# Two-way attention and two expert layers on one core: where the side work stands in a step of TensorE

## The chip, the cores and the metric

The kernel runs on one core of a Trainium2 chip. Its time is the device time of one execution in microseconds (us); lower is better. A median over several executions is given, and one more execution was profiled.

## What is computed

```python
# attention: x (8,8,512,64), state (8,8,32,64), batch and head first
a = softmax(scale * x @ state.T);  xread = a @ state
a2 = softmax(scale * state @ x.T); sread = a2 @ x
x = concat([xread, sread], axis=2)        # -> (4352, 512) rows
# first layer, w_in (512,2048), w_out (2048,512)
h = x @ w_in
x = (h - tanh(h)) @ w_out
# second layer, 8 experts, each token goes to its best one, w1 (8,512,1024), w2 (8,1024,512)
probs = softmax(x @ w_gate);  e = argmax
out[token] = probs[e] * (relu(x[token] @ w1[e]) @ w2[e])
```

## The kernel before

**The dense part.** The function `attention_moe_kernel` runs over 9 tiles t: one of 512 rows for each of the B = 8 batches (the xread rows), and a last one of 256 rows (all the sread rows). Each tile has FC = 16 chunks f of the 2048 hidden columns. A step c = 16 t + f on TensorE is: `first_product(c)`, the product h of chunk c, which writes one of two PSUM banks; `second_product(c - LAG)` with LAG = 3, the product with w_out that adds the chunk of three steps ago into the four banks of x2 (one for each 128 rows); and `side_work(c)`. All products are split in a high and a low part of the operands, so h takes 6 matmuls of 512 columns (r and three pairs of parts), and the product of x2 takes 12 (four blocks of rows, three pairs of parts). Nearly all matmuls are issued by the helper `mm` on line 1002, so the rows of the trace tell them apart by their operands: `ps<-A,G` is h, `ps<-wout,g_hi` and `ps<-wout,g_lo` are the product of x2, `ps<-win,stT` is `make_G`.

The text calls the side work of step f "side f", and the end of the h product of step f "the end of h f".

**The side work** is what the next tiles need and what the last tile leaves: 
- side 0: `turn_sread` and, from tile 2 on, `ranks(t - 2)`. 
- sides 1 to 3: `make_G`, the quarters 1 to 3 of G = state times w_in of this tile, which the h products of f = 4 on read. Side 1 waits for `ranks_read` from tile 2 on.
- sides 4 to 6: `turn`, `turn` and `gate_logits` of the tile before; side 7: `turn_logits`.
- sides 7 to 11: `attn_stage(t + 1, 0..4)`, side 12: `make_G(t + 1, 0)`, sides 13 to 15: `attn_stage(t + 1, 5..7)`. Only where a tile t + 1 below 8 follows, so 7 times.

Each side stage writes the two PSUM banks P0 and P1 (called P01 together). ScalarE (ACT) copies them out, for G also VectorE (DVE) takes the low part from them (`make_G_lo`, line 815), and the next side stage waits for that.

**The other engines.** Each of them has an order written out by hand, by step. ACT in step c: `tanh_of(c)` (lines 599 to 601, three passes over h), `g_hi_of(c - 1)` (line 607), in step 2 `y_copies` of the four x2 banks of the last tile (line 624), and then its share of the side work (such as `make_G_hi`, line 588). DVE in step c: `h_less_tanh(c)` (lines 897, 901, 904, 906), then its share. GpSimd (POOL) makes `g_lo` (line 480), and in steps 12 and 13 runs `shift` (line 451) and `normalize` (line 456) ahead of the `g_lo` of its own step. All wait in order: nothing passes a waiting instruction on its engine.

**The chain of the state softmax.** In tile t, for tile t + 1: side 11 writes the scores, ACT copies them (`S1_copied`), DVE takes the maxima (`max_states`), POOL subtracts them (`shift`, in step 12 behind `g_lo` of chunk 11), ACT takes the exponential (`exp_states`, line 577), DVE sums (`sums`), POOL multiplies (`normalize`, in step 13 behind `g_lo` of chunk 12), and then side 14 (`attn_stage(t + 1, 6)`, line 1046) turns the result on TensorE; it waits for `a_ready`.

The semaphore of h chunk c is waited for by ACT; h c + 2 waits for `g_made` of chunk c, since it takes its bank.

**Behind the dense part** comes the table of tokens by expert and a loop over tiles of 128 tokens, each with its expert's weights. The change doesn't touch it.

Of the kernel before, what the change touches and what calls it, by code (L numbers as in the profile page):

```python
# [21 lines left out]
def attention_moe_kernel(nc, x, state, w_in, w_out, w_gate, w1, w2, out):  # L22
# [50 lines left out]
    with ExitStack() as ctx:  # L73
# [244 lines left out]
        def width(t):  # L318
            return S if t < B else SR
# [680 lines left out]
        def _(pe):  # L1000
            def mm(o, l, r, start, stop):
                return nc.tensor.matmul(o, l, r, start=start, stop=stop)  # L1002
# [56 lines left out]
            def make_G(b, nb):  # L1059

                for pr in range(PAIRS):
                    for r in range(2):
                        rows = slice(D * r, D * (r + 1))
                        last = mm(ps[NS * pr:NS * (pr + 1), 6 + r, :], stT[rows, pr, NS * r:NS * (r + 1)],
                                  win[rows, pr, nb * 512:(nb + 1) * 512], True, True)
                last.then_inc(G_done, 1)

            def turn_sread(b):
                pe.wait_ge(sreadN_made, b + 1)
                nc.tensor.transpose(P0[:, 0:P], sreadN[:].rearrange("p r d -> p (r d)"), ident[:]).then_inc(sread_turned, 1)  # L1070

            def turn(t, i):
                pe.wait_ge(y_copied, C * t + i + 1)
                for k in range(K):
                    last = nc.tensor.transpose(ps[:, 6 + i % 2, P * k:P * (k + 1)], x2[:, i, P * k:P * (k + 1)], ident[:])  # L1075
                last.then_inc(x2_turned, 1)

            def gate_logits(t):

                pe.wait_ge(x2T_copied, C * (t + 1))  # L1080
                for k in range(K):
                    last = mm(P0[NS * k:NS * (k + 1), :], wg[:, k, :], x2T[:, :, k, :], True, True)
                last.then_inc(logits_done, 1)

            def turn_logits(t, bank, n):
                pe.wait_ge(LT_copied, t + 1)
                for i in range(n):
                    last = nc.tensor.transpose(bank[:, P * i:P * (i + 1)], LT[:, P * i:P * (i + 1)], ident[:])
                last.then_inc(LT_turned, 1)

            def ranks(tp, n):
                pe.wait_ge(onehot_made, tp + 1)
                mm(P1[:, 0:n * E], before[:], onehot[:, 0:n, :].rearrange("p t e -> p (t e)"), True, False)
                mm(P1[:, 0:n * E], ones[:], seen[:, 0:n, :].rearrange("p t e -> p (t e)"), False, True
                   ).then_inc(ranks_done, 1)

            def first_product(c):
                t, f = c // FC, c % FC
                if c >= 2:
                    pe.wait_ge(g_made, c - 1)  # L1100
                o = PH[c % 2][:, 0:width(t)]
                fs = slice(f * P, (f + 1) * P)
                if t < B:
                    if f == 0:
                        pe.wait_ge(A_lo_made, t + 1)
                    if f % 4 == 0:
                        pe.wait_ge(G_lo_made, NB * t + f // 4 + 1)
                    hi, lo = A_hi[t % 2], A_lo[t % 2]
                    for r in range(2):
                        for q, (l, m) in enumerate(((G_hi, hi), (G_hi, lo), (G_lo, hi))):  # L1110
                            last = mm(o, l[:, r, fs], m[:, r, :], r == 0 and q == 0, r == 1 and q == 2)
                else:
                    if f == 0:
                        pe.wait_ge(sread_copied, B)
                    for k in range(K):
                        last = mm(o, win[:, k, fs], sread[:, k, :], k == 0, k == K - 1)
                last.then_inc(h_done, 1)

            def second_product(c):
                t, f = c // FC, c % FC  # L1120
                n = width(t)
                pe.wait_ge(g_lo_made, c + 1)
                if t == 0 and f % 2 == 0:
                    wait_split(pe, f // 2)
                for i in range(n // P):
                    if f == 0 and t > 0:
                        pe.wait_ge(y_copied, C * (t - 1) + i + 1)
                    ts = slice(i * P, (i + 1) * P)
                    for q, (l, r) in enumerate(((g_hi, wout_hi), (g_hi, wout_lo), (g_lo, wout_hi))):
                        last = mm(PY[i], l[:, c % GR, ts], r[:, f, :], f == 0 and q == 0, f == FC - 1 and q == 2)  # L1130
                    if f == FC - 1:
                        last.then_inc(y_done, 1)
                if f < FC - 1:
                    last.then_inc(g_used, 1)
                else:
                    pe.sem_inc(g_used, 1)

            def side_work(c):
                t, f = c // FC, c % FC
                if f == 0:  # L1140
                    if t == 0:
                        attn_stage(0, 7)
                    elif t < B:
                        turn_sread(t)
                    if 2 <= t < B:
                        ranks(t - 2, C)
                elif f < NB and t < B:
                    if f == 1:
                        if t == 0:
                            pe.wait_ge(sreadN_made, 1)  # L1150
                        else:
                            pe.wait_ge(sread_copied, t + 1)
                        if t >= 2:
                            pe.wait_ge(ranks_read, t - 1)
                    else:
                        pe.wait_ge(G_lo_made, NB * t + f)
                    if t == 0:
                        pe.wait_ge(win_loaded[f], 16)
                    make_G(t, f)
                if t == 0 and f == 5:  # L1160
                    pe.wait_ge(G_lo_made, NB)
                    turn_sread(0)
                if t > 0:
                    if f == 4:
                        if t < B:
                            pe.wait_ge(G_lo_made, NB * (t + 1))
                        else:
                            pe.wait_ge(ranks_read, t - 1)
                            pe.wait_ge(logits_made, t - 1)
                        turn(t - 1, 0)  # L1170
                        turn(t - 1, 1)
                    elif f == 5:
                        for i in (2, 3):
                            pe.wait_ge(x2T_copied, C * (t - 1) + i - 1)
                            turn(t - 1, i)
                    elif f == 6:
                        gate_logits(t - 1)
                    elif f == 7:
                        turn_logits(t - 1, P1, C)
                if f == 11 and t >= B - 1:  # L1180
                    pe.wait_ge(logits_made, t)
                    ranks(t - 1, C)
                if t + 1 < B:
                    if f == 7 and t == 0:
                        pe.wait_ge(sread_copied, 1)
                    if f == 8 and t > 0:
                        pe.wait_ge(logits_made, t)
                    if 7 <= f < 12:
                        attn_stage(t + 1, f - 7)
                    elif f == 12:  # L1190
                        pe.wait_ge(S1_copied, t + 2)
                        make_G(t + 1, 0)
                    elif f > 12:
                        attn_stage(t + 1, f - 8)
# [17 lines left out]
            pe.wait_ge(gate_w_loaded, 16)  # L1212
            for c in range(FC * (B + 1)):
                first_product(c)
                if c >= LAG:
                    second_product(c - LAG)
                side_work(c)
            for c in range(FC * (B + 1) - LAG, FC * (B + 1)):
                second_product(c)

# [113 lines left out]
```

## Time and profile before

| | before |
|---|---|
| median of 3 executions | 1280.41 us |
| lowest, highest | 1278.49, 1280.99 us |
| the profiled execution, its own time | 1278.91 us |
| its span | 1277.2 us |
| mean granted TensorE clock | 0.978 |
| busy: TensorE matmul (and weight loads), ACT, DVE, POOL | 95% (75%), 50%, 58%, 41% |
| busy time of TensorE matmul | 1213.2 us |

The span runs from the first to the last instruction of the profiled execution; its own time lies 1.7 us above it. The share of busy time is an average: the dense part takes the stretch from about 40 us to 750 us, the experts that from about 798 us to the end.

### The profile page before, as it was taken

How to read it: one execution, taken by the hardware profiler on the slowest of the kernel's cores; microseconds unless marked ns; L12 is line 12 of the kernel's file. 1: busy time of each engine (PE TensorE's matmuls, PEld its weight loads, DVE VectorE, ACT ScalarE, POOL GpSimd, SP SyncE). 2: the span in 40 equal slices, each digit the busy share in tenths (PEclk: the TensorE clock that was granted, in tenths of full speed). 3: DMA queues.
4: the chain of work that ended last, by engine and by line, in shares of the span. 5: the costliest groups of instructions: out<-in, count | busy, mean ns of one | idle time of the engine just before them, and what ended most of it. 6: DMA issues, size and time to landing. Idle time of an engine off the chain costs nothing.

```text
span 1277.2 us, 20438 instructions
## 1 busy us (share of the span) xinstructions
PE 1213.2 (95%) x6740; PEld 961.1 (75%) x6741; DVE 745.3 (58%) x1018; ACT 632.8 (50%) x1088; POOL 522.3 (41%) x379
## 2 busy tenths in 40 slices
PE   6799999999999999999999965999999999999995
PEld 4577777877777777777778744888888888888884
DVE  4698788788887888878887765050500023282400
ACT  3556666666665666566654532333333333333332
POOL 3244234244243442434424232454544455555543
PEclk8899999999999999999999987999999999999998
DMA  8200301103003020020200206142411123353311
GB/s 261 67 20 1 67 3 47 23 1 67 3 9 61 1 67 3 1 67 1 77 24 4 96 18 222 42 133 82 141 66 41 41 89 123 113 168 102 104 35 37
DMA packets 74655, 80.71 MB, mean 63 GB/s; under 512 B 52063, under 2 KB 52063, under 8 KB 73570
## 3 DMA queue, kind: packets, MB, share of 16 engines
q1 hardware_dynamic: 55506, 59.80, 16.3%
q0 software_dynamic: 7568, 20.03, 4.7%
q10 hardware_dynamic: 11520, 0.09, 0.5%
q8 instruction: 37, 0.61, 0.2%
q14 instruction: 24, 0.20, 0.1%
HBM read 61.70 MB, written 19.49 MB: 64 GB/s over the span
## 4 chain that ended last, share of the span: by engine, by line
PE 80%; DVE 6%; POOL 5%; ACT 3%; DMA 3%; issue 2%; ACTq 0%; POOLq 0%; SPq 0%; DVEq 0%
PE ps L1002 72%; PE ps L1281 3%; POOL g_lo L480 2%; PE ps L1244 1%; DMA sread<-x_rows,take 1%; POOL xx L456 1%; POOL xx L451 1%; PE ps L1075 1%; PE ps L1019 1%; DVE u L904 1%; DVE u L897 1%; PE ps L1046 1%; ACT th L600 1%; DMA take<-expert_tokens 1%; DVE u L901 1%
## 5 line engine op out<-in xcount | busy, mean ns | idle before, releaser
L1002 PE MATMUL ps<-W,A 128*128 x1872 | 448.6, 395 | 2.8 <-ACT A L715 1.3
L1002 PEld LDWEIGHTS ps<-W,A 128*128 128x128 f32 x1872 | 347.4, 189 | 73.5 <-issue 3.8
L480 POOL TENSOR_TENSOR g_lo<-u,g_hi 128x512 fp32r<-128x512 f32 (+1 forms) x144 | 186.8, 1297 | 435.7 <-ACT g_hi L607 404.2
L1002 PE MATMUL ps<-wout,g_hi 128*128 128x512 f32 x1088 | 339.2, 393 | 0.4 <-POOL g_lo L480 0.4
L1002 PEld LDWEIGHTS ps<-wout,g_hi 128*128 128x128 f32 x1088 | 204.2, 188 | 43.8 <-POOL g_lo L480 1.1
L1002 PE MATMUL ps<-A,G 128*128 128x512 f32 x768 | 210.3, 409 | 4.4 <-issue 2.5
L1002 PE MATMUL ps<-wout,g_lo 128*128 128x512 f32 x544 | 212.4, 390 | 0.0
L889 DVE CAST W<-xn 128x1024 fp32r<-128x1024 f32 x28 | 21.5, 769 | 303.6 <-PE ps L1002 302.7
L904 DVE COPY_PREDICATED u<-big,th 128x512 f32<-128x512 uint8 (+1 forms) x144 | 179.7, 1248 | 23.4 <-DVE u L901 23.1
L1002 PEld LDWEIGHTS ps<-A,G 128*128 128x128 f32 x768 | 135.7, 189 | 67.9 <-issue 39.8
L599 ACT ACTIVATE u<-ps 128x512 f32<-128x512 f32 (+1 forms) x144 | 82.7, 574 | 118.1 <-PE ps L1002 97.9
L897 DVE SCALAR_TENSOR_TENSOR u<-u 128x512 f32<-128x512 f32 (+1 forms) x144 | 109.8, 763 | 48.8 <-ACT u L599 48.8
L1002 PEld LDWEIGHTS ps<-wout,g_lo 128*128 128x128 f32 x544 | 102.1, 188 | 22.3
L709 ACT ACTIVATE th<-ps 128x1024 f32<-128x1024 f32 x39 | 40.0, 1027 | 142.2 <-PE ps L1002 142.2
L901 DVE SCALAR_TENSOR_TENSOR u<-u,ps 128x512 f32<-128x512 f32 (+1 forms) x144 | 94.8, 658 | 24.0 <-ACT big L601 14.1
L721 ACT ACTIVATE sread<-ps,put 128x512 f32<-128x512 f32 x39 | 26.8, 687 | 159.3 <-PE ps L1002 150.9
L501 POOL TENSOR_TENSOR A<-LT,A 128x512 fp32r<-128x512 f32 x40 | 54.3, 1358 | 122.1 <-ACT LT L705 122.1
L506 POOL TENSOR_TENSOR A<-u,A 128x1024 fp32r<-128x1024 f32 x39 | 97.8, 2509 | 4.6 <-ACT u L716 4.0
L906 DVE TENSOR_TENSOR u<-ps,u 128x512 f32<-128x512 f32 (+1 forms) x144 | 95.3, 662 | 4.9
L607 ACT CAST g_hi<-u 128x512 fp32r<-128x512 f32 (+1 forms) x144 | 87.5, 608 | 7.2 <-DVE u L906 7.2
L495 POOL DMA_INDIRECT out_rows<-sread,put x39 | 47.1, 1208 | 100.4 <-ACT sread L721 96.0
L601 ACT ACTIVATE big<-ps 128x512 uint8<-128x512 f32 (+1 forms) x144 | 83.3, 579 | 0.0
(154 smaller groups left out, 1211.9 us busy)
## 6 DMA issues: line engine op xcount, KB each, us to landing
xn<-in_moe_w SPq DMA_DIRECT2D x32, 512.0 KB
xn<-in_x SPq DMA_DIRECT2D x32, 256.0 KB
x_rows<-xx SPq DMA_DIRECT2D x8, 1024.0 KB
spare<-in_moe_w SPq DMA_DIRECT2D x16, 512.0 KB
sp<-in_moe_w SPq DMA_DIRECT2D x16, 512.0 KB
win<-in_moe_w_in SPq DMA_DIRECT2D x4, 1024.0 KB, 11.2
Araw<-in_moe_w_out SPq DMA_DIRECT2D x6, 512.0 KB, 6.2
spare<-in_moe_w_out SPq DMA_DIRECT2D x2, 512.0 KB, 6.0
```

The source lines that it names most:

```text
L480: nc.gpsimd.tensor_tensor(g_lo[:, c % GR, 0:n], u[:, c % 2, 0:n], g_hi[:, c % GR, 0:n], ALU.subtract).then_inc(g_lo_made, 1)
L495: nc.gpsimd.indirect_dma_start(out, bass.IndirectOffsetOnAxis(ap=put[:, 0:1], axis=0), y_rows, None, bounds_check=TOK - 1, oob_is_err=Fals ...
L501: nc.gpsimd.tensor_tensor(xe_lo.rearrange("p k s -> p (k s)"), xe_raw, xe_hi.rearrange("p k s -> p (k s)"), ALU.subtract).then_inc(xe_lo_m ...
L506: nc.gpsimd.tensor_tensor(he_lo.rearrange("p k s -> p (k s)"), h_raw, he_hi.rearrange("p k s -> p (k s)"), ALU.subtract).then_inc(he_lo_ma ...
L599: nc.scalar.activation(u[:, c % 2, 0:n], h, ACT.Square, scale=SQ ** 0.5).then_inc(v_made, 1)
L601: nc.scalar.activation(big[:, c % 2, 0:n], h, ACT.Square, scale=0.5 ** 0.5 / SMALL).then_inc(big_made, 1)
L607: nc.scalar.copy(g_hi[:, c % GR, 0:n], u[:, c % 2, 0:n]).then_inc(g_hi_made, 1)
L897: nc.vector.scalar_tensor_tensor(uu, uu, LIN, uu, ALU.add, ALU.mult).then_inc(poly_made, 1)
L901: nc.vector.scalar_tensor_tensor(uu, uu, 1.0, h, ALU.add, ALU.mult).then_inc(near_made, 1)
L904: nc.vector.copy_predicated(uu, big[:, c % 2, 0:n], tt).then_inc(tanh_chosen, 1)
L906: nc.vector.tensor_tensor(uu, h, uu, ALU.subtract).then_inc(g_made, 1)
L1002: return nc.tensor.matmul(o, l, r, start=start, stop=stop)
```

## The change

In the loop over the steps on TensorE, `side_work(c)` is called between `first_product(c)` and `second_product(c - LAG)`, no longer behind both.

```diff
             for c in range(FC * (B + 1)):
                 first_product(c)
+                side_work(c)
                 if c >= LAG:
                     second_product(c - LAG)
-                side_work(c)
             for c in range(FC * (B + 1) - LAG, FC * (B + 1)):
                 second_product(c)
```

The orders of ACT, DVE, POOL and SyncE stay word for word as they are, and so do the number of instructions and what each waits for. Two places of the order on TensorE show what moves. `xx` holds the state softmax, `A` and `G` are the operands of h, `wout`, `g_hi` and `g_lo` those of the product of x2. First, step 14 of a tile, before:

```order
L1002 MATMUL ps<-A,G 128x512 [waits g_made]
L1002 MATMUL ps<-A,G 128x512 x5
L1002 MATMUL ps<-wout,g_hi 128x512 [waits g_lo_made]
...
L1002 MATMUL ps<-wout,g_lo 128x512
L1046 MATMUL ps<-ident,xx 128x128 [waits a2T_copied,a_ready]
L1046 MATMUL ps<-ident,xx 128x128 x7
```

And with the change:

```order
L1002 MATMUL ps<-A,G 128x512 [waits g_made]
L1002 MATMUL ps<-A,G 128x512 x5
L1046 MATMUL ps<-ident,xx 128x128 [waits a2T_copied,a_ready]
L1046 MATMUL ps<-ident,xx 128x128 x7
L1002 MATMUL ps<-wout,g_hi 128x512 [waits g_lo_made]
...
L1002 MATMUL ps<-wout,g_lo 128x512
```

The 12 matmuls of the product of x2 have gone from ahead of side 14 to behind it; between side 13 and side 14 there is still one product of x2, that of the step before.

Second, step 3 of a tile, before, with the wait for the four copied banks of x2 and the one for the last quarter of G:

```order
L1002 MATMUL ps<-A,G 128x512 x5
L1002 MATMUL ps<-wout,g_hi 128x512 [waits y_copied,g_lo_made]
L1002 MATMUL ps<-wout,g_hi 128x512
...
L1002 MATMUL ps<-wout,g_lo 128x512
L1002 MATMUL ps<-win,stT 32x512 [waits G_lo_made]
L1002 MATMUL ps<-win,stT 32x512 x7
```

And with the change:

```order
L1002 MATMUL ps<-A,G 128x512 x5
L1002 MATMUL ps<-win,stT 32x512 [waits G_lo_made]
L1002 MATMUL ps<-win,stT 32x512 x7
L1002 MATMUL ps<-wout,g_hi 128x512 [waits y_copied,g_lo_made]
L1002 MATMUL ps<-wout,g_hi 128x512
...
L1002 MATMUL ps<-wout,g_lo 128x512
```

In step 2 the same move puts the last product into the x2 banks of the old tile, for which ACT's `y_copies` wait, behind `make_G` of quarter 2.

## Rows read from the trace of the kernel before

**Rows 1.** Busy time by stretch: length, then PE, PEld, DVE, ACT, POOL, clock, DMA.

```profile
45.00:90.00 45.00, 39.99 (x214) 29.64 (x214) 40.97 (x45) 26.77 (x51) 18.98 (x11) 1.00 0.21 49
...
289.00:371.00 82.00, 81.84 (x509) 62.36 (x508) 68.41 (x99) 51.99 (x96) 30.50 (x22) 1.00 0.14 27
...
687.00:750.00 63.00, 61.57 (x290) 50.77 (x290) 44.29 (x93) 30.83 (x82) 19.30 (x23) 1.00 0.15 51
```

**Rows 2.** Timeline of TensorE, tile 3, step 14: start, length, instruction, idle before.

```profile
356.84 0.61 PE L1002 MATMUL ps<-wout,g_hi 128*128 128x512 f32 x2
...
359.33 0.39 PE L1002 MATMUL ps<-wout,g_lo 128*128 128x512 f32 x1
359.88 1.09 PE L1046 MATMUL ps<-ident,xx 128*128 128x128 f32 x8 [0.16 <-POOL xx L456]
```

**Rows 3.** Who waited for line 456, us in total and times.

```profile
  PEld ps L1046: 4.1, 7
```

**Rows 4.** Timeline of POOL, tile 3, steps 12 to 14.

```profile
350.19 2.38 POOL L451 TENSOR_TENSOR xx<-xx,m 128x1024 f32<-128x1024 f32 x1
355.77 1.72 POOL L480 TENSOR_TENSOR g_lo<-u,g_hi 128x512 fp32r<-128x512 f32 x1 [3.20 <-ACT g_hi L607]
357.43 2.40 POOL L456 TENSOR_TENSOR xx<-xx,r 128x1024 f32<-128x1024 f32 x1
```

**Rows 5.** Timeline of ACT, tile 3, steps 12 and 13.

```profile
346.73 0.60 ACT L599 ACTIVATE u<-ps 128x512 f32<-128x512 f32 x1 [0.36 <-PE ps L1002]
...
352.60 1.06 ACT L577 ACTIVATE xx<-xx 128x1024 f32<-128x1024 f32 x1 [1.05 <-POOL xx L451]
353.57 0.58 ACT L599 ACTIVATE u<-ps 128x512 f32<-128x512 f32 x1
...
355.00 0.63 ACT L607 CAST g_hi<-u 128x512 fp32r<-128x512 f32 x1
```

**Rows 6.** Timeline of TensorE, tile 1, steps 2 and 3.

```profile
133.19 0.39 PE L1002 MATMUL ps<-wout,g_lo 128*128 128x512 f32 x1
133.51 1.09 PE L1002 MATMUL ps<-win,stT 64*32 64x512 f32 x16
...
138.85 1.09 PE L1002 MATMUL ps<-win,stT 64*32 64x512 f32 x16
```

**Rows 7.** Timeline of ACT, tile 1, step 2.

```profile
132.84 2.07 ACT L624 COPY xx<-ps 128x512 f32<-128x512 f32 x4
134.75 1.08 ACT L588 CAST G<-ps 128x1024 fp32r<-128x1024 f32 x1
```

**Rows 8.** Timeline of DVE, tile 1, step 2.

```profile
135.86 1.23 DVE L815 TENSOR_TENSOR G<-ps,G 128x1024 fp32r<-128x1024 f32 x1
```

**Rows 9.** Timeline of TensorE, tile 3, sides 1, 8 and 13.

```profile
292.77 1.09 PE L1002 MATMUL ps<-win,stT 64*32 64x512 f32 x16
...
328.96 1.04 PE L1019 MATMUL ps<-ident,xn 128*128 128x128 f32 x8
...
354.59 1.03 PE L1040 MATMUL ps<-ident,xx 128*128 128x128 f32 x8
```

**Rows 10.** Timeline of DVE, tile 3: what sides 1, 8 and 13 wait for.

```profile
291.09 0.19 DVE L875 TENSOR_TENSOR score<-ps,region 128x32 f32<-128x32 f32 x1
...
326.19 0.28 DVE L829 TENSOR_REDUCE logits<-ps 128x32 f32<-128x128 f32 x1
...
351.58 1.23 DVE L815 TENSOR_TENSOR G<-ps,G 128x1024 fp32r<-128x1024 f32 x1
```

**Rows 11.** Timeline of TensorE, first tile.

```profile
52.44 1.09 PE L1002 MATMUL ps<-win,stT 64*32 64x512 f32 x16 [3.27 <-DVE G L815]
...
57.77 1.09 PE L1002 MATMUL ps<-win,stT 64*32 64x512 f32 x16
...
76.76 1.67 PE L1002 MATMUL ps<-A,G 128*128 128x512 f32 x6 [0.76 <-DVE u L906]
```

**Rows 12.** Timeline of DVE, first tile, steps 2 and 3.

```profile
56.34 1.22 DVE L815 TENSOR_TENSOR G<-ps,G 128x1024 fp32r<-128x1024 f32 x1
```

## The prediction

> **What bounds the kernel now.** I read four views, in this order. The page's busy time first (the table above): TensorE is busy for 95% of the span and loads weights for 75%. A share over all stages doesn't say what the dense part is worth, so next the busy time by stretch [rows 1]: in a full tile TensorE is busy 81.84 of 82.00 us, in the first tile 39.99 of 45.00 and in the last 61.57 of 63.00. So from 45 to 750 us it sits idle for some 5.0 + 1.4 us in the first and last tile and 0.16 in each of the eight stretches between (1.3): **7.7 us in all**. No order can win more than that there, since the change takes no instruction away. What it can lose is open: each side stage waits for ACT, DVE or POOL, and these waits are hidden now only because they end before TensorE comes to the side. Hence the third view, the timelines around each side: when does what it waits for end, and what would be left if TensorE came sooner? The fourth, who waited for line 456, says which wait already isn't hidden: side 14 waited 7 times, 4.1 us in total on the weight loads [rows 3].
>
> **What moves.** The product of x2 lasts, from its first matmul at 356.84 to its last at 359.33, 11 spacings of 0.227 us; 12 of them are **2.73 us** [rows 2]. It goes from ahead of each side to behind it. From one side to the next the same work stands as before (one h, one product of x2), so nothing changes between sides. But what the sides wait for hangs on the ends of h (ACT's tanh passes come first in its step, then g_hi, DVE and POOL follow), and from the end of an h to a side of the same or a later step there is now one product of x2 less: every side comes 2.73 us sooner against those engines. A wait with slack over 2.73 us, or one that moves along with the side itself, costs nothing; one with slack s costs 2.73 - s; one with no slack costs all of it. Switching between kinds of matmul occurs as often as before (h, side, x2 for x2, side, h), and I cost it at nothing. The h products wait for g_made of two chunks ago; one side and one product of x2 lie in between as before.
>
> I went through all 16 sides of a full tile.
>
> *Side 14 (`a_ready`).* The h of step 12 ends just before 346.73, where ACT's tanh begins [rows 5]. From there to POOL's `shift` at 350.19 there is g_hi and g_lo of chunk 11 in between; `shift` takes 2.38 [rows 4], ACT's exponential stands at 352.60, tanh of step 13 follows at 353.57 and g_hi at 355.00 [rows 5], then POOL's g_lo from 355.77 and `normalize` from 357.43 to 359.83 [rows 4]. Side 14 starts at 359.88 [rows 2], 13.15 us behind the end of h 12. That whole chain is anchored to the end of h 12, and it is longer than what TensorE has to do, so it has no slack: it started 0.23 us later than the usual 0.32 behind the last matmul at 359.33 [rows 2]. Side 14 can't come sooner, and the product of x2 that covered the chain is now behind it. Full price: **2.73 us, 7 times, 19.1 us**. In this is what side 13 waits (its G low part ends at 352.81 [rows 10], side 13 would come at 354.59 - 2.73 = 351.86 [rows 9], so it waits 1.0): both lie ahead of the same fixed point.
>
> *Side 3 (`G_lo_made`).* In step 2 ACT copies the four x2 banks of the old tile, 132.84 to 134.91, and only then quarter 2 of G [rows 7]; DVE takes its low part from 135.86 to 137.09 [rows 8]; side 3 starts at 138.85 [rows 6], a slack of 1.7. Now the last of those banks is done after `make_G`. The end of h 2 is at about 130.84 (2.75 ahead of 133.58, where the last matmul of x2 ends [rows 6]); with the side, 1.11 us, ahead of it, the fourth bank is done at 134.69, its copy takes to about 135.25, the copy of G (1.02) to 136.2, DVE's low part (1.23) to 137.5. Side 3 would come at 138.85 - 2.73 = 136.12. It waits **1.42 us, in tiles 1 to 7: 9.9 us**. If ACT passed these on with no delay, its old time of 137.09 would give 1.0 each.
>
> *Side 1 (`ranks_read`).* DVE reads the ranks at the end of a row of small operations behind its step 0, to 291.28; side 1 starts at 292.77 and would come at 290.04 [rows 9, 10]. With 0.05 for the semaphore: **1.29 us, in tiles 2 to 7: 7.7 us**.
>
> *Side 8 (`logits_made`).* DVE ends the logits at 326.47, side 8 starts at 328.96 and would come at 326.23 [rows 9, 10]: **0.29 us, in tiles 1 to 6: 1.7 us**.
>
> *All others* wait for one ACT copy of the side before. ACT is through with tanh and g_hi some 2.1 us behind the end of h (353.57 to 355.63 [rows 5]) and then copies for 1.0, so it is done 3.2 us after the side began where a side comes every 5.0. Side 12 is the tightest, since ACT takes two exponentials ahead of its copy, by an estimated 0.3 us. Nothing. Side 2 and side 4 gain what sides 1 and 3 wait and stay just clear (0.4 us each). The store of x2 starts with the last copy, and the transposes' copies come as long after it as before: nothing.
>
> *First tile.* No product of x2 stands in steps 0 to 2, so nothing moves there. Side 3 waits for quarter 2's low part, which ends at 57.56 [rows 12]: it starts then, where it now starts at 57.77 [rows 11], but the product of x2 comes behind it, so h 4 is late by 2.5 us. Here DVE is the bound (40.97 busy of 45.00 [rows 1]) and takes up some 1.5 of that. Bounds: 0 (DVE and a DMA set the pace anyway, h 8 waits 0.76 for DVE [rows 11]) and 2.6. I take **1.4**. *Last tile and experts:* sides 4 to 7 and 11 only, with 3 us steps whose copies take under 2.5: nothing. The experts shift as a whole.
>
> **Sum:** 19.1 + 9.9 + 7.7 + 1.7 + 1.4 = 39.8 us. On the profiled execution's own 1278.9 this is 1318.7. The median of the runs shown is 1.5 above that execution, so I predict **1320.2 us**, 3.1% slower.
>
> **The rivals.**
> - *The chains come forward with the sides (faster).* The Trainium skill, Perfetto Trace Analysis, Optimization Strategy, says to find the gap on the engine that matters and to make what it waits for start sooner; this change does start every side stage sooner. As a mechanism: the copies fall in ACT's idle time, POOL's `shift` starts early enough that side 14 no longer waits (0.23 us, 7 times), and the first tile's h products no longer wait for DVE (0.76 and two smaller, 1.7 in all): -3.3 us, 1277.1. It decides if `shift` begins before 350.19 minus 0.23 relative to h 12. Against it: `shift` stands behind g_lo of chunk 11, which hangs on the end of h 12 and not on side 11. 2%. That it all cancels, within 0.2%: 2%.
> - *Only the wait without slack pays.* Sides 1, 3 and 8 depend on sums of durations that DVE and POOL stretch or shorten. If those stay hidden: 19.1 and nothing else, 1299.5. Against it are the slacks of 1.5 to 2.5 in the rows. 9%.
> - *The waits add instead of overlapping.* Side 13's 1.0 us comes on top of side 14's 7 times, and the first tile pays 2.6: 39.8 + 7.0 + 1.2, 1328.4. For it: POOL and DVE hold each other up now and then (g_lo takes 1.72 instead of 1.3 [rows 4]). 11%.
> - *The clock falls after the new waits.* The granted clock was 0.978 on average, so somewhere in the run, outside the dense stretches, it was at the lower of its two levels. If each wait at side 14 cost the next h and x2 (4.1 us) half their speed: 7 more times 4.1, 28.7, 1349. Against it: side 2 of the first tile came after 3.27 us idle and still took 1.09, as everywhere, with a clock of 1.00 in that stretch [rows 1, 11]; only the one at side 3 of the first tile (2.6) is longer than 2.0. [...] 2%.
>
> **How the numbers follow.** The forecast has 74%. The range reaches from just above the case where only side 14 pays to just above the one where waits add: 1304 to 1330, which leaves out the ends, some 15%. What a measurement of this kernel can tell from no change is about 0.2%, 2.6 us. Slower by more: 74 + 9 + 11 + 2 = 96%. Within it 2%, faster 2%.
>
> **What would show it.** In the new profile: side 14 (line 1046) waits for POOL line 456 some 2 us, 7 times, side 13 some 1 us for DVE line 815; `make_G` waits for line 815 in step 3 by some 1.4 us in tiles 1 to 7 and for line 875 in step 1 by 1.3 us in tiles 2 to 7; side 8 waits some 0.3 us for line 829. The busy time of TensorE stays at 1213 us, its clock at 0.98, the tiles 2 to 6 each get 5.7 us longer (2.73 + 1.42 + 1.29 + 0.29), and the experts take as long as now. Tiles no longer than now would prove me wrong: then the chains follow the sides and not the h products. Tiles over 8 us longer would mean a wait that I put down as hidden.

## The result, and the profile after

The changed kernel takes 1325.93 us in the median of 4 executions (1323.43 to 1328.79), the kernel before 1280.12 us beside it. The ratio is 1.036, 95% interval 1.0334 to 1.0387: slower by 45.8 us. The forecast was 1320.2, slower by 39.8.

| | before | after |
|---|---|---|
| the profiled execution, its own time | 1278.91 us | 1323.43 us |
| its span | 1277.2 us | 1321.7 us |
| mean granted TensorE clock | 0.978 | 0.976 |
| busy time of TensorE matmul | 1213.2 us | 1220.1 us |
| share of TensorE, ACT, DVE, POOL | 95, 50, 58, 41% | 92, 47, 57, 39% |

The list of who waited for whom, TensorE alone, in the changed kernel: us in total, times, longest.

```profile
PE ps L1002 <- DVE G L815: 14.1, 9, 3.4
PE ps L1046 <- POOL xx L456: 13.0, 7, 1.9
PE ps L1040 <- DVE G L815: 10.9, 8, 5.2
PE ps L1002 <- DVE score L875: 8.0, 6, 1.3
...
PE ps L1019 <- DVE logits L829: 0.9, 6, 0.2
```

Five sides wait, and they are those of the forecast: sides 3, 14, 13, 1 and 8. Of the nine waits of the first row one was there before (3.35 us, side 2 of the first tile) and one is new and small (0.35 us, side 3 of the first tile); of the eight of the third one was there before (5.2 us, at the start). The timeline of TensorE, between side 13 of tile 2 and side 3 of tile 3, answers to [rows 2, 6, 9]:

```profile
281.98 1.06 PE L1040 MATMUL ps<-ident,xx 128*128 128x128 f32 x8 [0.81 <-DVE G L815]
...
289.02 1.09 PE L1046 MATMUL ps<-ident,xx 128*128 128x128 f32 x8 [1.87 <-POOL xx L456]
...
302.76 1.52 PE L1002 MATMUL ps<-A,G 128*128 128x512 f32 x6
305.61 1.09 PE L1002 MATMUL ps<-win,stT 64*32 64x512 f32 x16 [1.33 <-DVE score L875]
...
309.50 1.52 PE L1002 MATMUL ps<-A,G 128*128 128x512 f32 x6
310.95 1.09 PE L1002 MATMUL ps<-win,stT 64*32 64x512 f32 x16
...
314.84 1.52 PE L1002 MATMUL ps<-A,G 128*128 128x512 f32 x6
317.86 1.09 PE L1002 MATMUL ps<-win,stT 64*32 64x512 f32 x16 [1.49 <-DVE G L815]
```

From side 14 of one tile to side 14 of the next it is 88.35 us here (200.67 to 289.02), where it was 82.30 before (195.29 to 277.59, the same tile): 6.05 us more, and 5.99 to 6.07 in four of the five tiles 2 to 6. That the waits are those of fixed chains is to be seen on POOL, in the same tile:

```profile
278.09 1.30 POOL L480 TENSOR_TENSOR g_lo<-u,g_hi 128x512 fp32r<-128x512 f32 x1 [3.67 <-ACT g_hi L607]
279.34 2.38 POOL L451 TENSOR_TENSOR xx<-xx,m 128x1024 f32<-128x1024 f32 x1
284.92 1.72 POOL L480 TENSOR_TENSOR g_lo<-u,g_hi 128x512 fp32r<-128x512 f32 x1 [3.20 <-ACT g_hi L607]
286.60 2.37 POOL L456 TENSOR_TENSOR xx<-xx,r 128x1024 f32<-128x1024 f32 x1
```

ACT begins tanh of step 12 at 275.87 there:

```profile
275.87 0.60 ACT L599 ACTIVATE u<-ps 128x512 f32<-128x512 f32 x1 [0.57 <-PE ps L1002]
```

Side 14 starts at 289.02, 13.15 us later, to the hundredth what it was [rows 2, 5]. `shift` and `normalize` start 3.47 and 10.73 us behind that tanh, where they started 3.46 and 10.70 behind it. Not one link moved by more than 0.03 us.

One tile is out of line. From side 14 of tile 3 (377.38) to that of tile 4 (467.28) it is 89.90 us. The 8 us behind the two, by stretch (length, then PE, PEld, DVE, ACT, POOL, clock, DMA):

```profile
377.38:385.38 8.00, 8.00 (x91) 6.68 (x92) 4.44 (x6) 2.43 (x5) 1.27 (x1) 0.79 0.00 0
467.28:475.28 8.00, 8.00 (x98) 6.59 (x99) 5.54 (x8) 3.78 (x8) 1.82 (x2) 1.00 0.01 2
```

Behind the wait of 1.85 us at 377.38 the clock was at 0.79 on average, at the lower level for part of the 8 us. The forecast had that as a rival with 2%.

### The profile page after: what moved, and what is told of

Same layout as the page of the kernel before. It is cut to its first block, busy times and chain, and to the rows that moved or that the text cites. A ratio compares the mean times of both kernels' runs of the same rounds, so it can differ in the third digit from the quotient of the medians.

```text
span 1321.7 us, 20438 instructions
## 1 busy us (share of the span) xinstructions
PE 1220.1 (92%) x6740; PEld 961.0 (73%) x6741; DVE 752.8 (57%) x1018; ACT 624.2 (47%) x1088; POOL 518.8 (39%) x379
## 4 chain that ended last, share of the span: by engine, by line
PE 76%; DVE 8%; POOL 5%; ACT 5%; issue 3%; DMA 3%; ACTq 0%; POOLq 0%; SPq 0%; DVEq 0%
PE ps L1002 68%; PE ps L1281 2%; DVE u L904 2%; POOL g_lo L480 2%; PE ps L1244 1%; ACT th L600 1%; POOL xx L451 1%; POOL xx L456 1%; DMA sread<-x_rows,take 1%; ACT big L601 1%; DVE u L901 1%; DVE u L906 1%; PE ps L1019 1%; PE ps L1075 1%; DVE G L815 1%
## 5 line engine op out<-in xcount | busy, mean ns | idle before, releaser
L480 POOL TENSOR_TENSOR g_lo<-u,g_hi 128x512 fp32r<-128x512 f32 (+1 forms) x144 | 182.9, 1270 | 483.7 <-ACT g_hi L607 467.2
L1002 PE MATMUL ps<-wout,g_hi 128*128 128x512 f32 x1088 | 351.8, 404 | 0.4 <-POOL g_lo L480 0.4
L1002 PEld LDWEIGHTS ps<-wout,g_hi 128*128 128x128 f32 x1088 | 195.6, 189 | 73.8 <-issue 36.1
L904 DVE COPY_PREDICATED u<-big,th 128x512 f32<-128x512 uint8 (+1 forms) x144 | 189.4, 1315 | 23.4 <-DVE u L901 23.2
L1002 PE MATMUL ps<-A,G 128*128 128x512 f32 x768 | 198.6, 394 | 3.0 <-issue 2.5
L1002 PEld LDWEIGHTS ps<-A,G 128*128 128x128 f32 x768 | 145.1, 190 | 37.3 <-issue 4.6
```

Of the source, the lines that this page charges most:

```text
L480: nc.gpsimd.tensor_tensor(g_lo[:, c % GR, 0:n], u[:, c % 2, 0:n], g_hi[:, c % GR, 0:n], ALU.subtract).then_inc(g_lo_made, 1)
L904: nc.vector.copy_predicated(uu, big[:, c % 2, 0:n], tt).then_inc(tanh_chosen, 1)
```

## The experiments

Two theories were open. By the one each wait is the distance between a side and a chain that hangs on the ends of h. By the other the chains follow the sides, or the move costs by itself. And 6 us of the 45.8 were missing, for which the clock was a suspect. In all kernels below the times are set against the kernel before run beside them (1279.6, 1278.3 or 1279.0 us).

### Step 14 alone

```diff
+                t, f = c // FC, c % FC
+                early = f == 14
+                if early:
+                    side_work(c)
                 if c >= LAG:
                     second_product(c - LAG)
-                side_work(c)
+                if not early:
+                    side_work(c)
```

> Side work ahead of the product of x2 in step 14 alone (7 times), all else as before. Theory of the anchored chain (POOL's shift and normalize hang on the end of the h of step 12, not on the sides): side 14 can start no sooner than before, the product of x2 behind it is added in full, 7 x 2.73 = +19.1 us, 1299. Rival, the chains come forward with the sides: nothing here, since one side moved alone gives its producers nothing; it would say the same, so this run fixes the size and not the cause. Rival, the losses overlap with those of sides 1 and 3 in the changed kernel: then this alone would be over +25.

Measured: 1305.84 us (1301.79 to 1309.03), ratio 1.0192 (1.0162 to 1.0221), +26.3. That is 7 over the sum. The stretches of 8 us behind the first four of the seven sides 14:

```profile
113.58:121.58 8.00, 8.00 (x32) 6.64 (x33) 4.32 (x6) 2.17 (x4) 1.63 (x1) 0.79 0.00 0
199.68:207.68 8.00, 8.00 (x33) 6.85 (x34) 4.41 (x6) 2.18 (x4) 1.62 (x1) 0.79 0.00 0
286.17:294.17 8.00, 8.00 (x47) 6.53 (x51) 5.50 (x8) 3.09 (x5) 2.17 (x2) 1.00 0.00 0
371.15:379.15 8.00, 8.00 (x27) 6.70 (x28) 3.88 (x5) 1.01 (x1) 1.63 (x1) 0.62 0.00 0
```

In five of seven the clock fell (two at 0.62, three at 0.79). The two tiles that began at the full clock (286.17 to 371.15 is one) took 84.98 us, 2.68 more than 82.30; those with a fallen clock took 86.1 to 87.8, which is 1.5 to 2.8 us more than they would have. The wait is 2.85 us in one piece here, since side 13 doesn't wait. So the 2.73 us are right and the surplus goes with the clock; whether as its cause is the next experiment's to say. The row of side 14 itself tells cases apart: behind waits of the same length its eight transposes take 1.09 us at 286.17 and 1.97 at 371.15:

```profile
286.17 1.09 PE L1046 MATMUL ps<-ident,xx 128*128 128x128 f32 x8 [2.85 <-POOL xx L456]
...
371.15 1.97 PE L1046 MATMUL ps<-ident,xx 128*128 128x128 f32 x8 [2.85 <-POOL xx L456]
```

The profiled execution is the slowest of the four (1309.03 us), so it shows more of the clock than the median does.

### The wait filled with work, with step 14 alone and with the whole change

These lines are put into the kernel of step 14 alone, and with 16 in place of 22 into the changed kernel.

```diff
                     elif f > 12:
+                        if f == 14:
+                            pe.wait_ge(a2T_copied, t + 2)
+                            for i in range(22):
+                                nc.tensor.transpose(P0[:, P * (i % 4):P * (i % 4 + 1)], ident[:], ident[:])
                         attn_stage(t + 1, f - 8)
```

> Step 14 alone moved, and 22 transposes of the identity in its wait. Without them it took +26.3 us where 19.1 was expected; its trace has tiles of 84.98 us (82.30 + 2.68) with the clock at 1.00 and tiles of 86.1 to 87.8 with the clock at 0.62 to 0.88 behind side 14. Theory of the clock: filled, every tile takes 85.0 and the whole is +19, 1298 to 1299. Rival, the extra time is something else, say a refill of the weights behind the wait: still +26.

> The changed kernel with 16 transposes of the identity ahead of side 14, behind the wait for a2T_copied: they fill most of the wait of 1.85 us with work that nothing needs. The trace of the changed kernel has one tile of six that took 89.90 us instead of 88.3, with the clock at 0.79 in the 8 us behind side 14. If the idle time there brings the clock down in some tiles of some executions, the filled kernel loses these: 1 to 4 us less than the changed kernel's 1325.9 and a narrower spread. If only the wait itself counts, no change; if the transposes run over the end of the wait, up to +1.

Step 14 alone, filled: 1299.32 us (1298.29 to 1300.56), ratio 1.0161 (1.0142 to 1.018), +20.3 instead of +26.3. The whole change, filled: 1321.42 us (1319.52 to 1323.49), ratio 1.0329 (1.0311 to 1.0347), +42.4 instead of +45.8. (The two medians are 4.5 us apart, but the kernel before was 1.1 us faster beside the filled one.) Work was added and none left out, and neither became slower: step 14 alone became faster, its four executions all below the four unfilled ones; with the whole change the 3.4 us are near the scatter. The timeline of step 14 alone, filled, tile 1, and the 8 us from there:

```profile
194.51 2.57 PE L1197 MATMUL ps<-ident 128*128 128x128 f32 x22
197.53 1.09 PE L1046 MATMUL ps<-ident,xx 128*128 128x128 f32 x8 [0.46 <-POOL xx L456]
```

```profile
199.00:207.00 8.00, 8.00 (x95) 6.42 (x94) 5.70 (x7) 3.19 (x7) 1.46 (x2) 1.00 0.01 2
```

From side 14 to side 14 all tiles 2 to 6 take 84.96 to 85.02 us there, and 88.37 to 88.40 in the whole change, filled; the clock reads 1.00 behind all seven sides 14 of both. Each side 14 starts where it did, so the wait isn't shorter, it is only filled. The confidence intervals of the ratios of filled and unfilled overlap a little in both pairs; it is the tiles of the traces, all alike with the filling and, without it, longer behind every fallen clock, that decide.

### Step 3, steps 2 and 3, step 1

```diff
+                early = f == 3 and t > 0          # or: f in (2, 3) and t > 0
+                                                  # or: f == 1 and t > 1
```

> Side work ahead of the product of x2 in step 3 alone, tiles 1 to 7. Step 2 stays, so ACT copies the x2 banks as early as before and quarter 2 of G is ready at 137.1 in tile 1, where side 3 would come at 136.1: 7 x 1.0 to 1.1 = +7 to +8 us. If the whole of the changed kernel's wait at side 3 (1.49 in its trace) came from step 3's own move, +10.5.

> Side work ahead of the product of x2 in steps 2 and 3, tiles 1 to 7. Now the last product into the old x2 banks stands behind side 2, ACT copies them later and quarter 2 of G with them: 7 x 1.5 = +10.5 to 11 us, 3 us more than step 3 alone. If the banks' late copies don't matter, the same as step 3 alone; side 2 alone could cost at most 0.4 of a microsecond a tile.

> Side work ahead of the product of x2 in step 1 alone, tiles 2 to 7. DVE's reading of the ranks hangs on the end of the h of step 0: 6 x 1.4 = +8.4 us (1.29 by my sum, 1.33 of idle time in the changed kernel's trace and 0.07 of lost overlap). Rival, a move of a single side is absorbed by the slack of the next: under +3.

Step 3 alone: 1286.81 us, ratio 1.0057 (1.0039 to 1.0075), +7.2; each of the tiles 2 to 6 83.30 us, 1.00 more. Step 1 alone: 1287.66 us, ratio 1.0064 (1.0047 to 1.008), +8.1; each tile 83.7, 1.4 more. Both as expected. Side 3 of tile 3 in the kernel of step 3 alone:

```profile
303.78 1.09 PE L1002 MATMUL ps<-win,stT 64*32 64x512 f32 x16 [0.96 <-DVE G L815]
```

Steps 2 and 3: 1297.34 us, ratio 1.0138 (1.0111 to 1.0165), +17.7, well over the 11 expected. Its timeline of TensorE, tile 3, tells why:

```profile
301.16 1.09 PE L1002 MATMUL ps<-win,stT 64*32 64x512 f32 x16 [0.85 <-DVE G L815]
...
308.09 1.09 PE L1002 MATMUL ps<-win,stT 64*32 64x512 f32 x16 [1.49 <-DVE G L815]
```

The wait at side 3 is 1.49 us, as in the whole change, against 0.96 with step 3 alone: the late x2 banks are worth the difference (ACT's four copies of them take 2.67 us here, since they wait for banks in between, and 2.08 with step 3 alone). But side 2 waits too. Between side 1, which stayed behind its product, and side 2, which didn't, only one h is left. That is a fault of the experiment, not of the theory: an order that changes in the middle brings two sides close to each other, which the whole change never does.

### All steps but the five that wait

```diff
+                early = f not in (1, 3, 8, 13, 14)
```

> The new order in all steps but 1, 3, 8, 13 and 14, which stay as before. The theory says that sides 1, 3, 8, 13 and 14 carry all of the loss in the full tiles: within 2 us of before, with no more waits in tiles 1 to 7 than before. Rival, the move itself costs (switches between kinds of matmul, lost overlap): some 11 moved sides x 8 tiles x 0.1 = +9 us. Side 11 moved too, so the scores come 2.73 us sooner: if the chain of the state softmax hung on the sides, side 14 would stop waiting (0.16 of idle time now), -1.6 us.

Measured: 1306.78 us, ratio 1.0236 (1.0219 to 1.0253), +28.5. Wrong by all of it, for the same reason: the order changes at steps 2, 4, 9 and 15. The list of waits of TensorE:

```profile
PE ps L1002 <- DVE A L811: 11.7, 7, 1.7
PE ps L1002 <- DVE G L815: 8.9, 8, 3.0
PE ps L1075 <- DVE G L815: 6.4, 7, 0.9
```

New waits stand at side 15 (line 811, 1.67 us 7 times), side 2 (0.85) and side 4 (0.93), each the first early side behind a late one. It doesn't tell the theories apart, so it was done again with steps chosen for it.

### Only steps whose waits leave room

```diff
+                early = f in (5, 6, 7, 9, 10, 11, 12) and t > 0
```

> The new order in steps 5, 6, 7 and 9 to 12 of tiles 1 to 7 only: sides for whose waits the trace leaves room, and which follow an old side without a wait that binds (side 5 on the first copy of side 4, side 9 on one copy with 0.1 us to spare). If a move costs nothing by itself: within 1.5 us of before. Side 11, where the chain of the state softmax begins, comes 2.73 us sooner here while side 14 stays where it was: if that chain hung on the side, the delay of 0.23 us at side 14 would go, -1.6; if it hangs on the h of step 12, it stays at 0.16 of idle time.

Measured: 1280.25 us (10 executions), ratio 1.0003 (0.9989 to 1.0017). From side 14 to side 14 it is 82.30 to 82.32 us, as before. Seven sides a tile moved and none costs anything. And side 11 comes 2.73 us sooner, but side 14 still waits for POOL:

```profile
361.08 1.09 PE L1046 MATMUL ps<-ident,xx 128*128 128x128 f32 x8 [0.18 <-POOL xx L456]
```

So the chain doesn't follow the side where it begins.

### The first tile alone

```diff
+                early = t == 0 and f < 13
```

> The new order in the first tile alone, steps 0 to 12. By the sum +1.4 us (0 to 2.6); by the traces of the two kernels the first tile took 2.1 us more without the 2.73 of its side 14, part of it at a clock of 0.95: 0 to +2.1.

Measured: 1282.07 us, ratio 1.0028 (1.0012 to 1.0044), +3.8 with an interval from 1.5 to 5.6. That is above the 1.4 of the sum, but here, too, clock is mixed in. Side 2 of the first tile waits for some 3 us in every kernel. Behind that wait `make_G` took 1.96 us in 10 of the 14 profiled executions, and 1.09 in four, that of the kernel before among them. Here it is:

```profile
51.06 1.96 PE L1002 MATMUL ps<-win,stT 64*32 64x512 f32 x16 [3.36 <-DVE G L815]
```

From the first h to the start of side 14 it is 75.56 us here. Nine other kernels have the old order on TensorE up to there. In the three of them without a fall behind side 2 the same stretch takes 72.53 to 72.89 us (the kernel before 72.89), in the six with one 74.46 to 75.72. So the fall goes with some 1.6 to 3.2 us, and the 75.56 lie within what the old order takes with a fall: these single executions show no cost of the order in the first tile. Nor do they rule out the 1.4 of the sum. The 2.1 us by which the first tile of the changed kernel's trace is longer than before (75.02 against 72.89) may all be the clock's, since its side 2 had the fall and that of the trace before had not. The 3.8 us of the medians aren't explained.

### The shift one step sooner on POOL

```diff
-                    if f == 12:
+                    if f == 11:
                         shift(t + 1)
```

> The changed kernel with POOL's shift one step sooner, ahead of the low part of chunk 11 instead of behind it, so that it hangs on the maxima of DVE (347.7 in tile 3 of the trace before) and not on the end of the h of step 12 and a low part. Theory: the chain to side 14 comes some 2 us forward, the wait of 1.86 us there falls to 0.3 or less, side 13's wait of 0.82 for the low part of G stays, so 7 x 1.6 = 11 us less than the changed kernel, some 1314. Rival, the wait is bound by the sides or by something else on TensorE: no change, 1325.

> The kernel before with POOL's shift one step sooner. The only wait left in its full tiles is that of side 14, 0.16 of idle time and 0.23 us of delay, 7 times: -1.6 us, 1278.5, if nothing new waits. Rival: the low part of chunk 11 is 1 to 2 us later, which nothing needs for 10 us, or POOL and DVE hold each other up more: 0 to +2.

> The kernel before with POOL's shift one step sooner, once more and in more rounds: -1.6 us by the delay of 0.23 us at side 14, 7 times; the first time gave a ratio of 0.9986 (0.9975 to 0.9997).

In the changed kernel: 1312.76 us, ratio to the kernel before 1.0283 (1.0264 to 1.0302), +34.5 instead of +45.8: 11.3 us less, each set against the kernel before run beside it. The chain was cut at one link on POOL and the wait at side 14 is gone from the list; in its place side 15 waits for DVE:

```profile
PE ps L1040 <- DVE G L815: 10.9, 8, 6.1
...
PE ps L1002 <- DVE A L811: 5.5, 7, 0.8
```

A tile takes 87.26 us instead of 88.35, so 1.1 came back where I expected 1.6, since I had not looked at the low part of A behind side 14; 7.6 us in all. No side 14 of its trace is followed by a fallen clock, and the 3.4 us that the filling gave are likely the rest of the 11.3.

In the kernel before: 1276.76 us, ratio 0.9986 (0.9975 to 0.9997), 1.5 us faster, and again 1276.58 us, ratio 0.9981 (0.9971 to 0.9992), 2.4 us faster. From side 14 to side 14 it is 81.90 us instead of 82.30, and side 14 follows the product of x2 without a wait:

```profile
358.58 0.40 PE L1002 MATMUL ps<-wout,g_lo 128*128 128x512 f32 x1
358.82 1.04 PE L1046 MATMUL ps<-ident,xx 128*128 128x128 f32 x8
```

That is 0.40 us a tile and not 0.23. The 0.23 was taken against a gap of 0.32 us, which is the one ahead of `make_G`; ahead of a side of transposes that doesn't wait the gap is 0.23, in the trace before as here:

```profile
354.36 0.39 PE L1002 MATMUL ps<-wout,g_lo 128*128 128x512 f32 x1
354.59 1.03 PE L1040 MATMUL ps<-ident,xx 128*128 128x128 f32 x8
```

So side 14 was 0.32 us late before the change (359.88 less 359.33 is 0.55, less 0.23), and its row takes 1.04 us now where it took 1.09. This version is faster than both kernels, than the kernel before by 0.1 to 0.2%.

## Why the prediction was right, and where it was short

**The mechanism** held at every side. The waits were to be at sides 14, 13, 3, 1 and 8 and nowhere else in the full tiles, and they were. The time alone would not have shown it: 1325.9 is nearer to the 1328.4 of the rival by which the waits add than to 1320.2. By term, a tile:

| term | forecast | by the traces | alone |
|---|---|---|---|
| sides 13 and 14 | 2.73 | 0.81 + 1.87 of idle time, 0.16 before | 2.68, 2.70 filled |
| side 3 | 1.42 | 1.49 idle | (step 3 alone forecast 1.0: 1.00) |
| side 1 | 1.29 | 1.33 idle | 1.4 |
| side 8 | 0.29 | 0.15 idle | not run |
| a tile, 2 to 6 | 5.73 | 6.05 | |

The idle time of a row understates a wait by 0.07 us ahead of `make_G` and by some 0.15 ahead of transposes. Neighbouring matmuls overlap in the rows (0.39 us long, 0.227 apart), and behind a wait they don't. Counted from start to start, sides 1, 3 and 8 come 1.40, 1.57 and 0.31 us later behind their h than a side that doesn't wait (302.76 to 305.61 and 314.84 to 317.86, against the 1.45 of 309.50 to 310.95), where I had 1.29, 1.42 and 0.29. On side 1 it is the step from the producer's end to the side, which took 0.15 us (line 875 ended at 305.46) where I took 0.05; on side 3 the chain over the x2 banks was some 0.1 longer than my sum of its links. These are 0.28 us a tile more than the sum. Sides 13 and 14 give 2.66 where I had 2.73, so 0.07 less, and 0.11 isn't taken apart; together 0.32, the 6.05 less 5.73.

**The costs at nothing** were nothing: seven moved sides a tile gave a ratio of 1.0003 (0.9989 to 1.0017) and tiles as long as before. The forecast that the busy time of TensorE stays at 1213 us did not hold: it rose by 6.9. By an estimate from the figures above the overlap lost at sides 1, 3, 8 and 13 is some 3 us of that (0.07 to 0.16 each time); the rest wasn't taken apart, and the fallen clock is part of it.

**The term that was missing** is the clock, and the step behind it: "Against it: side 2 of the first tile came after 3.27 us idle and still took 1.09, as everywhere". One row of one execution was taken for a property of the chip. In 10 of the 14 profiled executions the clock was low behind that very wait. The rival came true in part: not 4.1 us behind each of seven waits but, in the profiled execution of the changed kernel, 1.6 us behind one. With the whole change the filling of the wait at side 14 gave back 3.4 us of the 45.8, with step 14 alone 6.0 of 26.3. I gave a fall 2% and no place in the sum. That it stayed small in the whole change, where the wait is 1.85 us in place of 2.85, I had not foreseen; for the number that was luck. The Trainium skill (TensorE: Matmul & The Clock Gate, Why this matters for your kernels) warns against idle gaps between bursts of matmuls in the middle of a kernel, but means longer ones than 1.85 us. The fall behind 377.38 came all the same, so here the measurement decides. The scatter of the times doesn't show the clock: it is 5.4 us over 4 executions of the changed kernel and 2.5 over 4 of the kernel before, but also 6.3 over 4 with steps 2 and 3 moved, where the clock reads 1.00 behind every side 14.

**The sum in the traces.** From the first h to the first row behind the dense part (line 1224) the profiled pair differs by 44.2 us, where the forecast's terms give 39.9. In the first tile it is 2.1 (forecast 1.4), from its side 14 to that of tile 6 36.4 (forecast 33.1, and the one fall is 1.6 of the difference), behind that 5.7 (forecast 5.4). The stretch behind the dense part took 1.7 us more and the one ahead of it 1.4 less; the order of the steps touches neither, and they nearly cancel. The filled kernel costs 42.4 by its median. How the 2.6 us over the sum divide is known only for the tiles: its trace has 35.1 us from side 14 to side 14 where the sum has 33.1.

**The other rivals.** Chains that come forward with the sides: refuted by step 11's move, which left side 14's wait where it was, and by the link of 13.15 us that the whole change left as it was. The Trainium skill's advice (Perfetto Trace Analysis, Optimization Strategy), to make what an engine waits for start sooner, was followed by the change only in name. What side 14 waits for is `normalize`, and the move that starts that sooner, `shift` on POOL, gave 11.3 us in the changed kernel and 1.5 and 2.4 in the kernel before. Only side 14 pays: refuted by steps 1 and 3 alone. The waits add: not so; side 13's 0.81 is taken off side 14's.

## What to carry to other kernels

Before side work is moved within a step, draw for each of its waits the chain back to the point on the same engine to which it is anchored; if the chain hangs on the main product and not on the side, moving the side forward by d costs d minus the slack, each time. Even a wait that shows only 0.16 us is a wait with no slack at all: it pays in full, and it is the place to look for a gain on the producers' engines. And moving single steps of a periodic order as an experiment changes the distance to their neighbours as well, so choose steps whose neighbours leave room.

## What the runs showed of the hardware

The granted clock of TensorE fell behind single waits of 1.9 to 3.4 us in an otherwise busy stretch, in some cases and not in others of the same kernel and execution: 5 of 7 waits of 2.85 us, 1 of 7 of 1.85 us, and 10 of 14 at side 2 of the first tile (all ten waits of 3.34 to 3.36 us; the four without a fall had 2.93, 2.96, 3.24 and 3.27, but the falls behind 1.85 and 2.85 us show that the length alone doesn't settle it). It fell behind none of 14 where transposes filled all but 0.46 us or less. A fall behind side 14 cost 1.5 to 2.8 us. Work that nothing needs, put into the waits of 2.85 us, made that kernel 6.0 us faster.
